# Near scores behind their masks, a two-part softmax, first sums on VectorE, first weights in eight pieces, rows stored late

## The reference

```
q_d, k_d, v_d = means over 4 positions            # [B, H, 144, 64]
out_up = repeat(softmax(scale * q_d @ k_d.T) @ v_d, 4)
mask = |i - j| < 4
out_local = softmax(where(mask, scale * q @ k.T, -1e9)) @ v
x = (out_up + out_local) as [B, S, H * D]
...
logits = x @ w_gate ; local = sigmoid(x @ w_local)
e = argmax(logits) if s == 0 or local < 0.5 else the expert of the token before
out = softmax(logits)[e] * (relu(x @ w1[e]) @ w2[e])
```

## Time and profile before

| what | value |
|---|---|
| median of 3 runs | 501.26 us (500.02 to 501.66) |
| the profiled execution | 502.7 us, with a span of 501.0 us |
| mean granted TensorE clock | 0.967 |
| PE, PEld busy | 462.3 us (92%), 371.0 us (74%) |
| DVE, ACT, POOL busy | 257.0, 217.3 and 192.7 us |
| PE's two expert products (L1405) | 134.3 and 133.9 us |

### The profile page before, as it was taken

The page is one execution under the profiler, slowest core; times in us unless marked ns, Lnnn a source line. Parts: engine busy times, 40 slices in busy tenths (PEclk is TensorE's granted clock), DMA queues, the critical chain, the costliest instruction groups (busy, mean ns, idle before and its releaser), DMA issues.

```text
span 501.0 us, 13091 instructions
## 1 busy us (share of the span) xinstructions
PE 462.3 (92%) x4156; PEld 371.0 (74%) x4163; DVE 257.0 (51%) x383; ACT 217.3 (43%) x377; POOL 192.7 (38%) x252
## 2 busy tenths in 40 slices
PE   7999999999889558999999999999999999999981
PEld 3787787788667325788888888888888888888860
DVE  3577777677556686353453452345346473522220
ACT  2666767767347220254244252525427282512220
POOL 7777677676459202113204213221321514042200
PEclk9999999999889867999999999999999999999997
DMA  8866665664966732215326421642646564121100
GB/s 179 171 151 161 174 159 149 172 155 92 353 175 149 253 122 43 22 44 211 139 90 230 146 82 48 211 153 78 211 156 231 170 245 156 69 73 35 36 26 6
DMA packets 85936, 69.22 MB, mean 138 GB/s; under 512 B 47886, under 2 KB 70926, under 8 KB 85904
## 3 DMA queue, kind: packets, MB, share of 16 engines
q1 hardware_dynamic: 81408, 57.78, 39.3%
q0 software_dynamic: 4496, 11.03, 7.1%
HBM read 59.34 MB, written 10.76 MB: 140 GB/s over the span
## 4 chain that ended last, share of the span: by engine, by line
PE 77%; DVE 9%; ACT 7%; issue 5%; POOL 1%; ACTq 0%; POOLq 0%; DVEq 0%
PE psum L1405 51%; PE psum L1423 4%; ACT early L656 4%; PE psum L1143 3%; PE psum L1126 3%; PE psum L1203 2%; DVE early L836 2%; DVE top_near L833 2%; PE psum L1179 2%; ACT early L671 2%; PE psum L1153 2%; PE psum L1383 2%; PE psum L1307 2%; PE psum L1317 1%; PE psum L1325 1%
## 5 line engine op out<-in xcount | busy, mean ns | idle before, releaser
L1405 PE MATMUL psum<-w_ring,xg_t 128*128 x552 | 133.9, 398 | 2.3 <-DVE xg_t L1065 1.6
L1405 PE MATMUL psum<-w_ring,h_t 128*128 x552 | 134.3, 398 | 1.9 <-issue 1.9
L1405 PEld LDWEIGHTS psum<-w_ring,xg_t 128*128 128x128 f32 x552 | 102.2, 188 | 25.0 <-issue 2.7
L1405 PEld LDWEIGHTS psum<-w_ring,h_t 128*128 128x128 f32 x552 | 102.0, 188 | 25.0 <-issue 2.4
L607 POOL DMA_INDIRECT out<-tile_bufs,to_row x23 | 23.5, 1024 | 197.3 <-DVE tile_bufs L1080 197.3
L1053 DVE TENSOR_TENSOR w_ring<-w_ring (+1 forms) x28 | 62.9, 2287 | 25.8 <-ACT w_ring L746 25.8
L767 ACT ACTIVATE tile_bufs<-psum 128x512 f32<-128x512 f32 x46 | 25.0, 596 | 86.9 <-PE psum L1405 86.8
L1065 DVE TENSOR_TENSOR xg_t<-psum,xg_t 128x512 fp32r<-128x512 f32 x24 | 16.5, 690 | 84.1 <-ACT xg_t L760 84.1
L746 ACT CAST w_ring<-w_ring (+1 forms) x28 | 52.1, 1910 | 17.4 <-DMA w_ring<-moe_w 17.4
L774 ACT CAST h_t<-psum 128x512 fp32r<-128x512 f32 x46 | 24.8, 591 | 76.3 <-PE psum L1423 76.2
L1080 DVE TENSOR_SCALAR tile_bufs<-psum,slot_w 128x512 f32<-128x512 f32 x23 | 17.2, 749 | 58.2 <-PE psum L1405 58.2
(11 more groups left out here) (179 smaller groups left out, 613.4 us busy)
## 6 DMA issues: line engine op xcount, KB each, us to landing
w_ring<-moe_w SPq DMA_DIRECT2D x16, 2048.0 KB, 9.1
early<-q SPq DMA_DIRECT2D x32, 144.0 KB, 2.5
early<-k SPq DMA_DIRECT2D x32, 144.0 KB, 3.1
early<-v SPq DMA_DIRECT2D x16, 288.0 KB
x_rows<-early SPq DMA_DIRECT2D x48, 96.0 KB, 2.5
early<-v SPq DMA_DIRECT2D x32, 120.0 KB
early<-v SPq DMA_DIRECT2D x64, 13.5 KB
early<-v SPq DMA_DIRECT2D x32, 15.0 KB
```

The costliest lines, as they stand in the source:

```text
L1405: ins = mm(bank[b][:, :], rows, w_ring[:, bass.ds(at + (off + c * width + n * 512), 512)], start=(c == 0 and k == 0), stop=(c == chunks - ...
```

## The change

It has five parts.

1. In every unit PE's `near_scores` comes directly behind `near_masked`, and `transposes(3)` behind it. The near softmax runs in two halves of three tiles: on DVE maximum, subtraction, maximum, subtraction over 324 columns each, on ACT one exponential a half, with the copies of `pool_out` for head 0 and 1 between them. On PE, `repeat(u - 1)` is cut in two and put ahead of each head's `pool_transposes`; `pool_values` goes head by head and waits for each head's copy; `near_transposes` waits for each half.
2. At the start 8 warm-up matmuls stand in place of 12, and 4, 4 and 2 + 2 later in place of 4, 6 and 6. The first transposes wait for q alone. DVE makes the sums of unit 0's q and k, behind its own copies. POOL builds `rep` directly behind the guards, and the wait for it has moved from before the loop into `repeat`.
3. Expert 0's weights are loaded in 8 pieces of 512 KB, two behind each two units in turns 2 to 5 of SP's loop.
4. `first_hi` 0 to 2 and `first_lo` 0 and 1 run in unit 15, and the others behind chunks 1, 8, 12 and 16.
5. The 48 stores wait for the last unit's `x_out`.

```diff
-    WARM, WARM_FIRST, WARM_TILES = 12, 6, 16
+    WARM, WARM_FIRST, WARM_TILES = 8, 4, 16
...
+            def load_first(i):
+                at = WCOLS + i * FCOL
+                if at < WCOLS + W1C:
+                    n = FCOL // F
+                    src, c, shape = w1v, i * n, dict(c=n)
+                else:
+                    n = FCOL // D
+                    src, c, shape = w2v, (at - WCOLS - W1C) // D, dict(c=n)
+                sp.dma_start(w_ring[:, at:at + FCOL].bitcast(F32).rearrange("p (c n) -> p c n", **shape),
+                             src[0, :, c:c + n, :]).then_inc(s_first_in, 16)
...
+            for kk in range(2, 2 + FPIECES // 2):
+                two_units(kk)
+                load_first(2 * kk - 4)
+                load_first(2 * kk - 3)
+            with sp.Fori(2 + FPIECES // 2, UNITS // 2) as kk:
...
-            load_w1(0)
-            load_w2(0)
+            sp.wait_ge(s_x, UNITS)
...
-                wait(sp, s_x, HP * (b + 1))
...
-            pool_qk(0, 0)
-            pool_v(0, 0, 0)
-            pool_qk(1, 1)
...
+            pool_v(0, 0, 0)
+            pool_qk(1, 1)
...
+            first_lo(0)
+            first_lo(1)
+            split_opool(UNITS - 1)
+            constants()
+            for i in range(2, FPIECES):
+                first_lo(i)
...
-            def exp_near(u):
-                wait(act, s_cenn, u + 1)
+            def exp_near(u, j):
+                tiles = slice(j * HALF, (j + 1) * HALF)
+                wait(act, s_cenn, 2 * u + j + 1)
                 wait(act, s_ptn, 2 * u)
-                nc.scalar.activation(p_near[:, :, :, 0:WIN].rearrange("p t h w -> p h t w"), cen_near[:],
+                nc.scalar.activation(p_near[:, tiles, :, 0:WIN].rearrange("p t h w -> p h t w"), cen_near[:, :, tiles],
                                      ACT.Exp, scale=SCALE).then_inc(s_expn, 1)
-            def pool_out(u):
+            def pool_out(u, h):
                 wait(act, s_opool, u)
-                for h in range(2):
-                    wait(act, s_ptp, 2 * u + h + 1)
-                    nc.scalar.copy(pt_pool[:, h, :], bank[TBANK[h]][0:PC + 1, 0:GW]).then_inc(s_ptp_out, 1)
+                wait(act, s_ptp, 2 * u + h + 1)
+                nc.scalar.copy(pt_pool[:, h, :], bank[TBANK[h]][0:PC + 1, 0:GW]).then_inc(s_ptp_out, 1)
...
+            def first_hi(i):
+                at = i * FCOL
+                act.wait_ge(s_first_in, 16 * FPIECES)
+                if i == 0:
+                    act.wait_ge(s_tr, 4 * UNITS)
+                elif i == 3:
+                    act.wait_ge(s_vpool, UNITS)
+                    act.wait_ge(s_pooled, 2 * UNITS)
+                elif i == 6:
+                    act.wait_ge(s_onear, UNITS)
+                nc.scalar.copy(w_ring[:, at:at + FCOL],
+                               w_ring[:, WCOLS + at:WCOLS + at + FCOL].bitcast(F32)).then_inc(s_first_hi, 1)
             def body(u, par, t=True):
                 if t:
                     tr_out(0, u + 1, 1 - par)
                     tr_out(1, u + 1, 1 - par)
+                else:
+                    first_hi(0)
                 exp_pool(u)
+                if not t:
+                    first_hi(1)
                 if t:
                     tr_out(2, u + 1, 1 - par)
                     tr_out(3, u + 1, 1 - par)
-                pool_out(u)
-                exp_near(u)
+                for j in range(2):
+                    pool_out(u, j)
+                    exp_near(u, j)
+                if not t:
+                    first_hi(2)
                 near_out(u)
...
-                if k % 3 == 2 and 4 <= k and k // 3 - 1 < FPIECES:
-                    first_hi(k // 3 - 1)
+                if k == 1:
+                    first_hi(3)
+                    first_hi(4)
+                elif k in (8, 12, 16):
+                    first_hi(k // 4 + 3)
...
-                wait(dve, s_cenn, u)
-                nc.vector.reduce_max(top_near[:], s4, X).then_inc(s_topn, 1)
-                wait(dve, s_topn, u + 1)
-                wait(dve, s_expn, u)
-                nc.vector.tensor_tensor(cen_near[:], s4, top_near[:].unsqueeze(3).broadcast_to([QP, 2, NT, WIN]),
-                                        ALU.subtract).then_inc(s_cenn, 1)
+                wait(dve, s_cenn, 2 * u)
+                wait(dve, s_expn, 2 * u)
+                for j in range(2):
+                    tiles = slice(j * HALF, (j + 1) * HALF)
+                    nc.vector.reduce_max(top_near[:, :, tiles], s4[:, :, tiles], X).then_inc(s_topn, 1)
+                    wait(dve, s_topn, 2 * u + j + 1)
+                    nc.vector.tensor_tensor(cen_near[:, :, tiles], s4[:, :, tiles],
+                                            top_near[:, :, tiles].unsqueeze(3).broadcast_to([QP, 2, HALF, WIN]),
+                                            ALU.subtract).then_inc(s_cenn, 1)
...
+            for a in range(2):
+                dve.wait_ge(s_tr_out, copied[2 * a + 1])
+                dve.wait_ge(s_tr_odd, a + 2)
+                t4 = qk_t[:, 0, a, :].rearrange("p (s r) -> p s r", r=POOL)
+                nc.vector.tensor_tensor(qk_part[:, a, :, :], t4[:, :, 0:2], t4[:, :, 2:4], ALU.add).then_inc(s_part, 1)
+                dve.wait_ge(s_part, a + 1)
+                nc.vector.tensor_tensor(qk_pool[:, 0, a, :], qk_part[:, a, :, 0], qk_part[:, a, :, 1],
+                                        ALU.add).then_inc(s_pooled, 1)
...
+                    wait(pe, s_q_in[par], 32 * (half + 1))
                     wait(pe, s_ptn_out, 2 * (u - 2) + g + 1)
                 else:
+                    wait(pe, s_k_in[par], 32 * (half + 1))
...
-                wait(pe, s_expn, u + 1)
                 for j in range(2):
+                    wait(pe, s_expn, 2 * u + 1 + j)
...
-                wait(pe, s_ptp_out, 2 * u + 2)
                 wait(pe, s_vpool, u + 1)
                 wait(pe, s_onear_out, u)
-                for qc in range(2):
-                    for h in range(2):
+                for h in range(2):
+                    wait(pe, s_ptp_out, 2 * u + 1 + h)
+                    for qc in range(2):
...
+            def repeat(u, first=0, end=HALF):
+                if first == 0:
+                    pe.wait_ge(s_reps, 1)
+                    wait(pe, s_osplit, 2 * u + 2)
+                    wait(pe, s_x, u)
+                for i in range(first, end):
...
+                near_scores(u, par)
                 if t:
                     transposes(3, u + 1, 1 - par, nxt)
-                near_scores(u, par)
-                pool_transposes(u, t)
-                if x:
-                    repeat(u - 1)
-                else:
-                    keep_warm(WARM_FIRST, 7)
+                for j in range(2):
+                    if x:
+                        repeat(u - 1, j, HALF if j else 1)
+                    else:
+                        keep_warm(WARM_FIRST // 2, 7)
+                    pool_transposes(u, j, t)
...
-            keep_warm(WARM_FIRST - 2, 7)
+            keep_warm(WARM_FIRST, 7)
             body(0, 0, 0, x=False)
-            pe.wait_ge(s_reps, 1)
```

69 lines of the change are left out of this document (25 added, 44 removed).

## The result

The changed kernel takes 498.51 us (median of 20 executions; 493.90 to 507.65), the one before 500.10 beside it: a ratio of 0.9948 with a 95% interval of 0.9923 to 0.9973. That is faster by 0.5%, against a forecast of 490.3 us (486.5 to 496). The profiled execution took 500.14 us with a span of 498.3.

What follows compares the result with a forecast made beforehand. The unit loop was taken as bound by PE's list, with gains only from its pauses. 4.6 + 2.8 + 3.6 = 11.0 us off the profiled 502.7 gives 491.7, so 490.3 for the median; range 486.5 to 496.

Steps and rivals of the forecast that it cites:

- They cost nothing: SP's loop: eight pieces add 0.5 MB a unit to 1.2 MB behind loads two units ahead, at no cost.
- part 1, the unit: Unit loop: removing two pauses on PE, less 0.08 for new joints, wins 0.33 a unit, 4.6 us over 14.
- part 2, the start: Start: fewer warm-ups, sums on DVE and no wait for `rep` win 2.8 us; bounds 1.3 and 3.5.
- parts 3 and 4, unit 15: Unit 15 and gate logits: no stop, no half clock and earlier splitting win 3.6 us; bounds 0.3 and 4.2.
- part 5, late stores: After the last `x_out`: 48 stores take 33.1 us, expert 1's cast keeps 5.8 us of cover, so no cost.
- the bound of 0.41: Unit loop: most a unit can win, 0.20 at the mask plus 0.21 waiting for ACT's near exponential; 5.7 us.
- the wait of up to 1.8 us: Start: DVE's sums could each wait for a POOL selection such as 0.46, leaving the start 1.0 instead of 2.8.
- Unit 15's stop: PE's 1.28 us idle amid unit 15's pooled values, taken as code coming late behind expert 0's loads, so it goes.
- The late stores: Rival: stores above 0.81 us each hold up expert 1's first tile; 502 to 504 at 1.05 each; chance 0.10.
- the clock at the start: Rival: fewer warm-ups may leave PE at the half clock through unit 0; about 493; chance 0.08.
- the loop's units: Rival: the unit loop does not shrink, the new chain of 3.51 being as long; price 4.6, 494.9; chance 0.12.
- the signs that were named for a wrong prediction: Units staying at 7.6, the clock falling in unit 15, or ACT waiting for expert 1's weights ahead of the first tile.

Runs made afterwards that it cites:

- e17: e1 with two extra 512 KB pieces, data unused, behind each of turns 2 to 5 of SP's loop, kept as a loop; 501.06 us.
- e2: The kernel before with only the changed kernel's SP loop, so the eight pieces in the loop; 505.28 us, ratio 1.0022.
- e15: e1, the same kernel, measured again in more rounds; 491.97 us, ratio 0.9816.
- e9: e1 with four of the eight pieces in SP's loop, two behind each of turns 2 and 3, the other four behind all loads; 496.19 us, ratio 0.9884.
- e4: The changed kernel with SP issuing one piece behind each unit instead of two behind each two units; 496.17 us, ratio 0.9892.
- e10: e1 with unit 9's q and k loads held until half of unit 7's near transposes, so q comes late; 501.73 us.
- e3: The changed kernel with the eight pieces issued from ScalarE's queue, one a unit in units 1 to 8, instead of SP's; 496.00 us, ratio 0.9905.
- e11: e10 with six warm-up matmuls on PE ahead of the wait for the late q; 498.15 us, ratio 0.9934.
- e12: The kernel before with expert 0's weight loads held until unit 15's pooled values are done; 502.06 us, ratio 1.0034.
- e6: e5 with the rows stored as before, each batch's 24 as soon as its own sums are there; 494.63 us.
- e8: e5 with the start of before: unit 0's sums on GpSimd and 12 and 6 warm-ups; 499.69 us.
- e1: The changed kernel with all eight pieces behind the last loads of v, first_hi and first_lo in their old places; 491.21 us, ratio 0.9813.
- e13: e1 with its pieces held until unit 15's pooled values are done and split behind chunks 9 to 23; 494.13 us, ratio 0.9861.
- e16: e1 with turns 2 to 5 of SP's loop written out, without a piece; 491.48 us.
- e14: e1 with turns 2 to 5 of SP's loop written out and two extra 64 KB pieces, data unused, behind each; 494.12 us.
- e18: e1 with two extra 64 KB pieces, data unused, behind each of turns 2 to 5 of SP's loop, kept as a loop; 491.91 us.
- e5: The changed kernel with its eight pieces between the last two loads of v's windows, early first_hi kept; 494.70 us, ratio 0.9884.

## Why the prediction was wrong

**The step that failed** is the sentence on the eight pieces: "They cost nothing", since the loads are "two units ahead" and the share of 0.63 plus some 0.2 leaves room. Both halves of it were wrong in the same way.
- *The share.* It is a mean over time in which SP also waits for PE. In the earlier trace rows SP's loads are paced by a unit of 7.64 us, 15.3 a turn. With part 1 the unit is 7.17, and as a loop SP's own turn through its 26 loads takes 13.7 us of the 14.34 that two units last. That leaves 0.65 us a turn, and a pair of pieces makes the turn 2.8 longer (e17). Written out, as in the changed kernel, SP has some 3 us to spare, but with pieces a turn takes 15.9 to 16.3 all the same. So each turn with pieces puts SP 1.5 to 2.4 us behind. Part 1 made this worse by 0.95 us a turn, which is nowhere in the prediction, but it is not what broke the step: about 16 us are above 15.3 too, and e2, with the old unit, has two turns of 16.7, a late k and no gain. Nor did the prediction ask what the share itself would become: it was 0.79 and 0.85 in the first two windows of e15's loop, with no piece in it, and 0.98 and 1.02 there with pieces.
- *The lead.* A buffer two units deep is not two units of cover. For the q awaited at 60.24, e15's issue ended at 53.56 + 0.83 = 54.39, and with its median landing of 2.5 us it was there 3.35 us early. In the changed kernel the issue ended at 58.00 (54.28 + 3.72), 3.6 later, and PE's wait ended 3.6 behind that, 1.1 more than the landing in e15. So of the 4.7 us by which q was later, 3.35 were covered and 1.36 are the wait. (The second 3.6 is read off the wait itself, so this divides the wait and doesn't test it.) Two turns with pieces were enough, as e9 shows alone.

```profile
49.73 1.38 SPq L374 DMA_DIRECT2D w_ring<-moe_w  x2
54.28 3.72 SPq L329 DMA_DIRECT2D early<-q  x2
```

- *The price.* The prediction put a lost cover at "at most a piece, 1.6 us" and at v. It was q, and behind a gap the clock fell. By the traces: 1.36 us of gap cost 3.2 us of unit in all, 2.24 cost 9.5, 2.11 in e9 cost 6.5, 2.42 in e17 9.8, 1.19 in e4 8.3, 1.05 in e2 7.6, 3.43 in e10 4.9. Gaps up to 1.24 us in e3 and 1.68 in e11 had no fall behind them. The fall is therefore worth nothing to 7.4 us, and I found no rule for its length. That it is why this kernel's executions spread from 493.9 to 507.7 is likely but not shown: the four longest have mean clocks of 0.938 to 0.947 and the four shortest of 0.960 to 0.969, but only one execution was profiled.

**What the other steps gave**, each by its own number, in the changed kernel's trace or in e15's where the pieces cover it:

| step | forecast | measured |
|---|---|---|
| part 1, the unit | 0.33 a unit, 4.6 us | 0.476 a unit, 6.7 us (107.02 to 100.34, e15) |
| part 2, the start | 2.8 us | 3.15 us (19.52 to 16.37) |
| parts 3 and 4, unit 15 | 3.6 us | 3.54 us (14.06 to 10.52), all of it the missing stop (10.35 in e12) |
| the pieces in the loop | 0 | -12.6 us (112.99 for 100.4) |
| part 5, late stores | 0 | 0 (e6; ACT waits for PE, not the weights) |

Part 1 was mis-sized because the bound of 0.41 counted only the two pauses that I had picked; the measured 0.476 is above it. The 6.7 us are even more than the 4.47 us for which PE was idle in the loop, so some 2.2 us of what the trace had as busy went too; matmul ends are modelled there, and I can't place them. The joints for which I took off 0.08 cost nothing visible. Part 2's 3.15 us are one pair of profiles. Unit 1's pooled scores started at 19.52 to 20.41 in the four profiles with the old start (before, e2, e8, e12) and at 15.79 to 17.16 in those with the new one, so its size is known to about 1 us either way. Part 2's sums on DVE cost as little as assumed: the first pooled scores start at 9.02, 0.4 ahead of the forecast, so the wait of up to 1.8 us that was weighed there didn't show. By the rule of the Trainium skill (SBUF — State Buffer, "Who interferes with whom") a sum with both inputs in SBUF could have waited for a selection of GpSimd's. In the changed kernel's trace the sum of 288 columns took 0.45 us both beside such a selection (at 7.46) and beside a constant fill (at 8.17), and that of 144 columns 0.31 both times, so no wait is seen. The selection reads only 8 columns, so this is a weak test.

In the sum the four parts give 13.4 us by unit 15's third chunk, minus 12.6: the trace has the third chunk at 139.88 for 140.60. The first expert product comes 2.24 us earlier (196.93 for 199.17), so 1.5 us more are won among the gate's chunks and the routing, whose parts I don't know. With the pieces behind, the third chunk of e15 is 12.8 us earlier and the first product 10.1, so 2.7 are given back there; in e1, the same kernel, 1.3. The routing runs at 0.5 to 0.84 of the clock in both, and five microseconds of e15's gate chunks (132.81 to 137.81) ran at 0.74, where e1's ran at 1.00.

**Unit 15's stop** was read rightly in kind. With the loads held it is gone, in the kernel before (e12, with nothing else changed) and in e1 (e13), so the traffic is needed for it. It is not sufficient: with the loads in flight it was 1.28 us before, 0.33 and 0.70 in the profiles of e1 and e15, 0.45, 0.60, 1.09 and 1.86 in e16, e10, e14 and e11, and not listed in e9, e17 and e18, whose pooled values took 1.61 us for the 1.40 of the changed kernel (e5 to e8 had PE waiting for ACT at that place). In the six kernels with nothing of expert 0 in flight there (the changed one, e2, e3, e4, e12, e13) it was never seen. That the late thing is PE's code, as the prediction took it, is still only argued; no run shows what was fetched. The Trainium skill (Runtime: NRT & Kernel Launch, "Instruction fetch mechanics") calls the fetch mostly hidden on straight code; these stops stand in straight code.

The rivals: none came true. The late stores were harmless at 0.68 us each, below the 0.81 from which they would have cost; the clock at the start held in the changed kernel's profile (in e10's and e16's, which start the same way, the first pooled scores ran at half the clock, 1.24 us for 0.71, and unit 1 came 0.8 us later); the loop's units shrank. What did happen, a late load in the loop, is neither among the rivals nor among the signs that were named for a wrong prediction. The time still came out slightly faster than before because the other terms gave 13.4 us where 11.0 were forecast.

## What to carry to other kernels

Ask of every queue how long its own pass takes against the pass of the engine that it feeds, and do so after the change that shortens the pass: a DMA share of 0.63 and a buffer two deep looked like room, but the queue's loop had 0.65 us to spare in 14.34, and with the two large loads a turn took about 16 us or more, as a loop and written out. When a transfer is not needed before a certain moment, put it behind the loads that are. And price a lost cover by what it triggers: where PE was the bound, gaps of 1 to 2.4 us cost from 3.2 to 9.8 where the clock fell behind them.

## What was not expected of the hardware

- Loads of 512 KB, issued by SP or by ScalarE, among packets mostly under 2 KB filled the 16 DMA engines at 200 to 220 GB/s (share 0.98 to 1.02 in the changed kernel, e3 and e4), while large loads nearly alone reached 395 GB/s (e5).
- Loads of 64 KB to 16 partitions took 5.8 us to land (e18), hardly less than those of 512 KB to 128 partitions in the same place (6.6, e17). The DMA share was 0.95 with them and 0.85 without (e15), at fewer GB/s (170 for 178), and SP's turns were some 1.3 us longer.
- The granted clock fell to 0.50 after gaps of 1.05 us (e2) and 1.19 (e4) and stayed at 1.00 after gaps of 1.24 and 1.68 us (e3, e11), and the fall lasted from some 3 us (e10) to some 17 (e2, e4). So the length of the gap alone did not tell what followed. Six warm-up matmuls in the gap went with a clock that stayed.
